# Mixer kernel on one core: plain blocks with units held in SBUF for the first supergroup

## What is computed

```python
q_s = exp(q - max(q, -1)); q_s /= sum(q_s, -1) + 1e-9
k_s = exp(k - max(k, 2));  k_s /= sum(k_s, 2) + 1e-9
x = q_s @ (k_s^T @ v)                    # to [8, 576, 512]
u = x + (relu(x^T @ w_tok1) @ w_tok2)^T
y = u + relu(u @ w_ch1) @ w_ch2          # first mixer, hidden 1536
xn = (y - mean(y)) / sqrt(var(y) + 1e-6) * g_ln
out = y + relu(xn @ w_ch1') @ w_ch2'     # second mixer, hidden 2048
```

## Time and profile before

| | us |
|---|---|
| median of 3 runs | 1565.05 (1563.29 to 1566.54) |
| profiled execution | 1563.69 |
| its span | 1561.9 |

### The profile page before, as it was taken

The page is one execution under the profiler, slowest core; times in us unless marked ns, Lnnn a source line. Parts: engine busy times, 40 slices in busy tenths (PEclk is TensorE's granted clock), DMA queues, the critical chain, the costliest instruction groups (busy, mean ns, idle before and its releaser), DMA issues.

```text
span 1561.9 us, 19837 instructions
## 1 busy us (share of the span) xinstructions
PE 1472.2 (94%) x7584; PEld 1322.4 (85%) x7584; DVE 1076.6 (69%) x1165; ACT 698.2 (45%) x844; POOL 309.0 (20%) x315
## 2 busy tenths in 40 slices
PE   6999896898999999899989999999999999999998
PEld 5988885787888887788878888888888888889998
DVE  7987876397486486496696687568657856872276
ACT  5656654352453453352452453344345424532342
POOL 6587785323303312300000000000000000000000
PEclk9999998899999999999999999999999999999999
DMA  7899985989989989979658767766876687667766
GB/s 241 256 306 296 299 282 202 403 318 366 354 291 379 372 294 362 352 288 317 240 184 300 248 209 266 249 247 219 275 243 228 237 277 244 211 219 256 251 214 199
DMA packets 150334, 429.28 MB, mean 275 GB/s; under 512 B 14240, under 2 KB 43488, under 8 KB 150240
## 3 DMA queue, kind: packets, MB, share of 16 engines
q1 hardware_dynamic: 132768, 361.94, 67.6%
q0 software_dynamic: 17472, 66.07, 11.8%
HBM read 348.26 MB, written 79.69 MB: 274 GB/s over the span
## 4 chain that ended last, share of the span: by engine, by line
PE 74%; DMA 10%; DVE 7%; issue 3%; SPq 2%; POOL 2%; ACT 2%; DVEq 0%; ACTq 0%; POOLq 0%
PE ps L1131 24%; PE ps L1133 23%; PE ps L1132 23%; DMA w_ring<-w_scratch_B 6%; DMA vt<-v 2%; SPq L289 2%; DMA qt<-q 1%; DVE o_lo L980 1%; DVE x_lo L834 1%; PE ps L1155 1%; DMA w_op<-w2b 1%; PE ps L1166 1%; DVE q_sum L761 1%; POOL q_lo L464 0%; DVE h L950 0%
## 5 line engine op out<-in xcount | busy, mean ns | idle before, releaser
L1131 PE MATMUL ps<-x_hi,w_ring 128*128 128x462 f32 (+1 forms) x980 | 369.2, 377 | 44.1 <-issue 15.1
L1131 PE MATMUL ps<-o_hi,w_ring 128*128 128x462 f32 (+1 forms) x980 | 367.4, 375 | 9.6 <-DVE o_lo L980 7.9
L1133 PE MATMUL ps<-x_hi,w_ring 128*128 128x462 f32 (+1 forms) x980 | 366.7, 374 | 0.0
L1132 PE MATMUL ps<-x_lo,w_ring 128*128 128x462 f32 (+1 forms) x980 | 366.7, 374 | 0.0
L1132 PE MATMUL ps<-o_lo,w_ring 128*128 128x462 f32 (+1 forms) x980 | 364.8, 372 | 0.0
L1133 PE MATMUL ps<-o_hi,w_ring 128*128 128x462 f32 (+1 forms) x980 | 364.6, 372 | 0.0
L671 ACT CAST o_hi<-h 128x924 fp32r<-128x924 f32 (+1 forms) x210 | 202.3, 963 | 254.8 <-PE ps L1133 225.0
L980 DVE TENSOR_TENSOR o_lo<-h,o_hi 128x924 fp32r<-128x924 f32 (+1 forms) x210 | 240.8, 1150 | 61.2 <-ACT o_hi L671 61.2
L1131 PEld LDWEIGHTS ps<-x_hi,w_ring 128*128 128x128 f32 x980 | 186.2, 190 | 74.3 <-issue 31.2
L1131 PEld LDWEIGHTS ps<-o_hi,w_ring 128*128 128x128 f32 x980 | 185.1, 189 | 40.1 <-issue 17.5
L950 DVE TENSOR_TENSOR h<-ps,h 128x924 f32<-128x924 f32 (+1 forms) x90 | 100.6, 1117 | 163.5 <-PE ps L1133 163.1
(11 more groups left out here) (140 smaller groups left out, 1831.3 us busy)
## 6 DMA issues: line engine op xcount, KB each, us to landing
w_ring<-w_scratch_C SPq DMA_DIRECT2D x280, 512.0 KB, 3.8
w_ring<-w_scratch_B SPq DMA_DIRECT2D x210, 512.0 KB, 5.6
w_scratch_C<-w_out POOLq DMA_DIRECT2D x8, 1792.0 KB, 11.7
w_scratch_C<-last_pair POOLq DMA_DIRECT2D x8, 1792.0 KB, 11.8
w_scratch_B<-w_out POOLq DMA_DIRECT2D x6, 1792.0 KB, 10.4
w_scratch_B<-last_pair POOLq DMA_DIRECT2D x6, 1792.0 KB, 9.9
kt<-kT SPq DMA_DIRECT2D x32, 288.0 KB, 6.0
u_scratch<-u_out SPq DMA_DIRECT2D x32, 288.0 KB, 3.8
```

Of the source, the lines that this page charges most:

```text
L1131: mm(dst, a_hi, b_hi, start=start, stop=False, skip_group_check=onto)
L1132: mm(dst, a_hi, b_lo, start=False, stop=False, skip_group_check=onto)
L1133: return mm(dst, a_lo, b_hi, start=False, stop=stop, skip_group_check=onto)
```

## The change

Position 0 no longer goes through `CALLS`. It is computed with plain blocks (eight products in place of seven) straight from the units that lie in SBUF: the raw blocks of a unit, with high and low part, are weights of position 0, and its four sums are made alongside and stored with them for the later positions. One raw block (the one that isn't among the seven operands) uses the last slot of the ring. TensorE works through 12 units of 48 matrix products: four groups of 12, each group with two PSUM banks. The takes, now with the relu in them, are on ScalarE after every second unit; the result is added at the end (`plain_add`). In the first stage no unit is made: two are loaded in steps 5 and 6, their raw parts cast at the end of steps 6 and 7. Low parts of all units are VectorE's. x of position 0 needs four pairs of parts and no sums. Ring entries are loaded from position 1 on. Units 13 to 27 are made at five entries in each of positions 1 to 3.

```diff
-    for pos in range(NX):
+    for pos in range(1, NX):
...
+    PLAIN = UNITS["B"]
+    HI_AT = {s * ENTRIES["B"] + e: PLAIN + 1 + 5 * s + i for s in range(3) for i, e in enumerate((0, 6, 11, 27, 36))}
...
+            w_out1 = sb("w_out1", [P, 7, 2, 2 * P], f32r, w)
...
+                if n == RW - 1:
+                    sp.wait_ge(groups, unit_over(PLAIN - 1))
...
-            for n in range(RW):
-                load_entry(n)
             step(NB - 1, 0)
             phase_a_over(sp)
+            for c in range(NC):
+                load_x(1, c)
+            for c in range(NC):
+                load_res(0, c)
+            for n in range(RW - 1):
+                load_entry(n)
+            for c in range(NC):
+                load_x(2, c)
+            store_plain(0)
+            store_plain(1)
+            load_entry(RW - 1)
+            store_plain(2)
+            store_plain(3)
...
                 if first:
                     sub_q(1, ST)
                     lo_q(1)
-                    load_unit(0)
                     return
-                load_unit(i)
+                if i in (NB - 3, NB - 2):
+                    load_unit(i - (NB - 3))
                 if later:
                     sub_q(i + 1, ST)
-                sum_unit(i - 1)
-                if later:
                     lo_q(i + 1)
-                lo_unit(i - 1)
-                store_unit(i - 1)
+                else:
+                    sum_unit(0)
+                    sum_unit(1)
...
+            for n in range(PLAIN):
+                if n >= 2:
+                    sum_unit(n)
+                store_unit(n)
+                load_unit(n + 2)
...
+            def hi_px(c):
+
+                if c == 0:
+                    act.wait_ge(kv_done, NB)
+                    act.wait_ge(x_in, 64)
+                n = 2 * SIZES[0]
+                nc.scalar.copy(plain_x(c)[0], xn[:, c * n:(c + 1) * n].rearrange("p (h n) -> p h n", h=2))\
+                  .then_inc(px_hi_made, 1)
+
+            def hi_raw(n):
+
+                act.wait_ge(wp_in[n % 2], 32 * (n // 2 + 1))
+                wait(act, wp_stored[n % 2], 16 * (n // 2))
+                if n >= 2:
+                    act.wait_ge(groups, unit_over(n - 2))
+                x = w_op[:, n % 2, :, :]
+                nc.scalar.copy(w_out[n % 2][:, 0, 0, :], x[:, 0, :]).then_inc(raw_hi_made, 1)
+                nc.scalar.copy(plain_w(n, 0, 1)[:, 0, :], x[:, 7, :]).then_inc(raw_hi_made, 1)
+                nc.scalar.copy(w_out[n % 2][:, 5:7, 0, :], x[:, 5:7, :]).then_inc(raw_hi_made, 1)
...
+            def plain(n):
+
+                if 2 <= n + 1 < PLAIN:
+                    hi_raw(n + 1)
+                if n < HC["B"]:
+                    if n % 2 == 1:
+                        plain_take(n, 0)
+                    hi_sums(n + 1)
+                    if n == 4:
+                        hi_po(0)
+                        hi_po(1)
+                    if n % 2 == 1:
+                        for g in range(1, NC):
+                            plain_take(n, g)
+                    return
+                r = 2 * (n - HC["B"]) + 2
+                if r < 2 * HC["B"]:
+                    hi_po(r)
+                if n + 1 < PLAIN:
+                    hi_sums(n + 1)
+                else:
+                    hi_unit(PLAIN)
+                if r < 2 * HC["B"]:
+                    hi_po(r + 1)
+                for p in {7: (0, 1), 8: (2, 3), 9: (4, 5), 10: (6,)}.get(n, ()):
+                    hi_x(1, p)
...
+            def plain_in(n):
+
+                pe.wait_ge(raw_lo_made, 3 * (n + 1))
+                if n == 0:
+                    pe.wait_ge(px_lo_made, NC)
+                for g in range(NC):
+                    if n == 0 and g == 1:
+                        pe.wait_ge(u_act, U_ACT * NB)
+                        pe.wait_ge(u_dve, U_DVE * NB)
+                    if n >= 2 and n % 2 == 0:
+                        pe.wait_ge(plain_relu, NC * (n // 2 - 1) + g + 1)
+                    for i in range(2):
+                        x = plain_product(plain_w(n, i, g // 2), g % 2, g, *plain_x(2 * i + n % 2),
+                                          n % 2 == 0 and i == 0, n % 2 == 1 and i == 1)
+                    x.then_inc(groups, 1)
...
+            for n in range(HC["B"]):
+                plain_in(n)
+            for n in range(HC["B"], PLAIN):
+                plain_out_of(n)
```

More of the change, by code:

```diff
@@ L624, in step @@
                             hi_q(i + 1, ST[c - 1:c])
-                    if later == 0 and c == 0:
-                        hi_x(0, 1)
+                    if later == 0 and c < 2:
+                        hi_px(2 + c)
                 if later:
                     hi_q(i + 1, ST[3:])
-                if later and not first:
-                    hi_unit(i - 1)
+                if later == 1:
+                    hi_raw(0)
+                    hi_raw(1)
             exp_q(0, ST)
@@ L691, in norm @@
                       .then_inc(root_made, 1)
-            hi_unit(NB - 2)
-            for p in (2, 3):
-                hi_x(0, p)
-            hi_unit(NB - 1)
+            hi_sums(0)
+            for n in range(PLAIN):
+                plain(n)
             for c in CALLS:
@@ new lines, in plain_add, with plain @@
+            def plain_add(g):
+                n = SIZES[0]
+                y = halves(res, n)[:, g, :, :]
+                if g == 0:
+                    dve.wait_ge(res_in, 64)
+                dve.wait_ge(groups, added(2 * HC["B"] - 1, g))
+                nc.vector.tensor_tensor(y, plain_group(g), y, ALU.add).then_inc(plain_out, 1)
+            def plain(n):
+                if 2 <= n + 1 < PLAIN:
+                    lo_raw(n + 1)
+                if n == 4:
+                    lo_po(0)
+                    lo_po(1)
+                r = 2 * (n - HC["B"]) + 2
+                if 2 <= r < 2 * HC["B"]:
+                    lo_po(r)
+                if n + 1 < PLAIN:
+                    lo_sums(n + 1)
+                else:
+                    lo_unit(PLAIN, 0)
+                    lo_unit(PLAIN, 1)
+                if 2 <= r < 2 * HC["B"]:
+                    lo_po(r + 1)
+                if n == 6:
+                    sum_x(1, 0)
+                if n == 7:
+                    lo_x(1, 0)
+                    lo_x(1, 1)
+                    sum_x(1, 1)
+                if n == 8:
+                    lo_x(1, 2)
+                    sum_x(1, 2)
+                    lo_x(1, 3)
+                if n == 9:
+                    lo_x(1, 4)
+                    lo_x(1, 5)
+                    sum_x(1, 3)
+                if n == 10:
+                    lo_x(1, 6)
@@ L941, in _ @@
             nc.vector.tensor_scalar(g_half[:, :], gcol[:, :], -0.5, None, ALU.mult).then_inc(ghalf_made, 1)
+            lo_sums(0)
+            for n in range(PLAIN):
+                plain(n)
+            for g in range(NC):
+                plain_add(g)
             def take(c, p):
```

177 lines of the change are left out of this document (118 added, 59 removed).

## The result

| | before | after |
|---|---|---|
| median of the runs | 1565.05 us (1559.63 to 1567.92) | 1555.24 us (1551.93 to 1557.58) |
| ratio | | 0.9948 (95% interval 0.9924 to 0.9972) |
| profiled execution, its span | 1563.69, 1561.9 | 1557.58, 1555.8 |

The changed kernel is faster by 0.5%, 9.8 us by the medians. The forecast was 20 us: the sign and the range held, the time that was named did not. The profiled execution of after is the slowest of its five; its gain over the profiled one of before is 6.1 us.

The account below looks back on a forecast made before the run. TensorE bounds the kernel (95% busy from 387 us), but position 0 loses time to waits and slow clock. Terms -5.0 + 0.6 - 20.5 + 2 + 1 + 2 + 1 = -18.9 took 1563.7 to 1544.8, given as 1545 us; range 1534 to 1557.

Parts of the forecast that it names:

- (1): Position 0's products: 576 plain ones at 0.2134 us take 122.9 us against 143.42, old waits gone: -20.5 us.
- (2): Start of position 0: last low part of x follows VectorE's copy, first product at about 244.1: +0.6 us (0 to +3).
- (3): Unit supply during position 0: a chain of up to 20.5 us is hidden; only the start is tight: +2 us (0 to 8).
- (4): VectorE in position 0: heaviest units hold 8.4 of 10.24 us, next x has slack: costed at nothing.
- the tight place: Start of position 0: unit 2, loaded from about 248.3, ready at 264 and wanted at 264.6; 2 us taken.
- rival D: Unit supply in position 0: 20 us from load issue to landing, 13.7 us a unit, whole slower at 1577 us; chance 0.07.
- Rivals B: Unit supply sets position 0 mildly: loads land only after stores, 12.0 us a unit, 1560 us (half effect 1552); chance 0.11.
- E: Start of position 0: first waits move rather than vanish if unit 2 comes 10 us late, 1555 us; chance 0.07.
- C: VectorE becomes position 0's bound, held up by GpSimd's sums: units 7 to 9 take 11.4 us, whole 1550; chance 0.05.
- (6): First stage without unit work: five steps come down to the 27.57 us one without a store: -5.0 us (0 to -10.7).
- rival A: First stage gains nothing: waits for v turn into waits for q's low part on GpSimd, 1550 us; chance 0.12.
- (5): Change to position 1 and after: late entry 3 +1, four y stores in position 1 +2, position 3's five units +1.

Follow-up runs that it names:

- a_work: Changed kernel with the units' sums, casts and low parts put back into its first stage, without their memory traffic: 1568.85 us, ratio 1.0006 to the kernel before.
- y_spread: Changed kernel with ring entry 3 ahead of position 0's y stores, which go one by one behind entries 5 to 8: 1553.28 us, 0.9901 of the kernel before.
- unit_late: Changed kernel with position 1's units made at entries 6, 11, 20, 27, 36 instead of 0, 6, 11, 27, 36: 1556.34 us, 0.9938 of the kernel before.
- y_late: Changed kernel with both y_spread's moved y stores and unit_late's later units: 1547.15 us, 0.9880 of the kernel before.
- b_nostore: Kernel before with the 1.8 MB stores of units 2 to 5 in first-stage steps 3 to 6 cut to 64 KB each: 1560.55 us, 0.9958.
- f1: y_spread with position 1's units at entries 5, 10, 15, 27, 36: 1548.91 us, 0.9891 of the kernel before.
- f2: As f1, but unit 12 moved to entry 3 of position 1 and the others at 8, 13, 18, 28, 37: 1551.58 us, 0.9877 of the kernel before.
- after_again: The changed kernel itself, unaltered, run once more on one chip with f1 and f2: 1556.30 us, 0.9916 of the kernel before.
- a_traffic: Changed kernel with the units' loads and 1.8 MB transfers put back into its first stage, without sums or casts: 1583.21 us, 1.0093 of the kernel before.

## Why the prediction was right or wrong

**(1) The products of position 0: right.** The sum had 122.9 us for 576 products. 355.02 - 228.28 = 126.74, less the waits of 2.73 at unit 2 and 1.09 at position 1, is 122.92. The pace of stage C held for plain blocks, the clock was 0.99, and the old waits of 10.18 and 7.82 us are gone, as forecast.

**(2) Start, (3) supply of units, (4) VectorE: right in size, except for a wait ahead of position 0.** The only wait inside position 0 is the one that was called the tight place, 2.73 us where 2 stood. Loads of units, from issue to landing, in the stretch 204 to 256 and then 256 to 345 us of after:

```profile
DMA to landing us min/median/max: 11.3/15.6/21.2
```

```profile
DMA to landing us min/median/max: 7.6/7.8/11.6
```

The load of unit 2 went out at 231.91, 3.6 us behind the first product (the sum had 4.2), and GpSimd's sums could start at 248.33: a landing of 16.4 us where 13.3 was the worst that the sum allowed. The sum had 0.6 us to spare there; the 3.1 us more of the landing, and casts and low parts of 3.1 us where it had 2.4, less the 0.6 by which the load went out earlier, come to about the 2.7. Unit 3's loads reached even the 20 us of rival D (19.8 and 21.2), but only they did: unit 4's took 11.3 to 11.6, unit 5's up to 8.7, the later ones 7.6 to 8.2. Rivals B and D, which needed slow landings in every unit, fell with that row, and so did E: unit 2 was late by 2.7 us, not 10. C fell too, though its premise held. By groups of VectorE's instructions in position 0 of after:

```profile
L967 DVE TENSOR_TENSOR w_out<-w_op,w_out 128x512 fp32r<-128x512 f32 x24 | 15.4, 686 | 15.9 <-ACT w_out L612 15.9
...
L961 DVE TENSOR_TENSOR w_out<-w_op,w_out 128x512 fp32r<-128x512 f32 x10 | 11.7, 1167 | 0.0
L959 DVE TENSOR_TENSOR w_ring<-w_op,w_ring 128x256 fp32r<-128x256 f32 x10 | 9.4, 942 | 0.0
L957 DVE TENSOR_TENSOR w_out<-w_op,w_out 128x256 fp32r<-128x256 f32 x10 | 7.7, 766 | 28.1 <-ACT w_out L606 28.1
```

The same 512 columns take 686 ns when GpSimd is done with its sums and 1167 when it sums beside them; 256 columns take 766 and 942 where the earlier trace rows has 0.42 us. The three raw parts of a unit cost 2.9 us, not 1.5. The Trainium skill (SBUF — State Buffer, Who interferes with whom) says that a VectorE instruction with two inputs in SBUF contends with a GpSimd instruction that reads SBUF; these rows agree in kind. But 1.4 us more a unit is half of the 3.0 of GpSimd's sums, which rival C added whole. Mostly this stayed hidden, with VectorE busy for 73.2 of 127 us, but not everywhere. At unit 2 the raw low parts took from 248.71 to 251.33, 2.6 us instead of 1.5, all of it in the chain that TensorE waited for: by estimate 1.1 us of the 2.7. And the sum of part (2) priced the raw parts of unit 0, in the last step but one, at nothing for VectorE: they took 3.6 us (204.02 to 207.57), a row of 512 columns 1.78, and TensorE then waited 2.40 us for qT_lo at 209.98, where the kernel before has such a wait of 1.20.

**(6) The first stage: right in sign, too small by a factor of three.** The first product came at 228.28, 15.3 us earlier; the sum had -5.0 + 0.6. The step that failed is the reference: "if the five steps come down to the one without a store". That step, 27.57 us, had no store, but it had the loads of two units, the four sums of one and its cast in it (the low parts followed at 80.91), and a DMA share of 0.84. It is not the step without a unit, which takes 25.69 us with TensorE busy for 127.13 of 128. Work (0.95) and stores (1.1 to 2.4) each had their price. The five steps that the sum counted took 207.50 - 76.58 = 130.92 us, 12.0 less than 142.88 where it had 5.0; the step ahead of them, which the sum left out, took 25.45 instead of 27.57, 2.1 less; and from the last k_den row to the first product it was 1.2 less where the sum had 0.6 more. The other reason was rival A's, which held the gain down: GpSimd's low part of q would be late next. But GpSimd had lost its own work, 68.06 us busy in 128 where it had been 112.87 in 144, and TensorE's wait for it was 0.7 us, once, against 5.2 in a_work, where that work is back. I priced the resource that was freed as though it were still loaded. Even the bound of -10.7 was passed, since it added up only waits that had been named in the stretch.

**(5) The change to position 1: wrong, and the largest error.** +3 us in the sum, up to 8.5 by its bounds, 14.8 measured. The parts were all seen: four y stores in position 1, entry 3 late behind two of them, a DMA share of 0.92. The step that failed is the price of the ring entries: each part was priced alone, the bytes at the position's mean rate and entry 3 by the 3.5 us wait that the kernel before has at this change. The store of unit 12 and of the unit of entry 0, which now fall there too, had no term. All of it falls into the same 25 us, at the one point where the ring has three entries and no more to follow. There the landing of an entry rose to 13.6 us against 7.7 us of work in the ring, and two waits with a stretch at clock 0.80 followed. y_spread, unit_late and y_late show that cause for the mixing-in half, 11.7 of the 14.8 us: either edit gives back a part, both give back the whole of that half. The other 3.1 us, in the mixing-out half, are no more than b_nostore has there (59.1 us) on the schedule of the kernel before.

**Positions 2 to 4.** Position 3 had +1; 118.2 and 115.1 against 113.6 contain it. The 4 us of position 2 weren't foreseen, came in both executions, and are unexplained: b_nostore, whose schedule there is that of the kernel before, has 118.2 as well.

**The sum.** The range held by luck. -15.3 and -16.7 against forecasts of -4.4 and -18.5 (its -20.5 and 2), then +14.8 against +3, and +11.0 in positions 2 to 4 (+5.5 in the second execution) against +1. The two large errors, 11 us too little gained and 12 too little given back, nearly cancel; what is left between 18.9 and the 6.1 us of the profiled executions is mostly positions 2 to 4, which no experiment explains.

**A better version.** The orders with the burst taken apart run at 0.988 to 0.989 of the kernel before (y_late, f1, f2), against 0.9948 and 0.9916 in the two measurements of the changed kernel. That both are beaten is likely, not shown: where they ran together the intervals still overlap, and in the profiled executions positions 1 to 3 together took 367.2 us in y_late, 364.2 in f1 and 362.3 in f2, against 366.5 in after and 363.2 in after_again. There position 2 was longer than in after (123.4, 122.5 and 120.7 against 118.9) by much of what position 1 had gained.

## What to carry to other kernels

When work leaves a stage, price what is left with everything of it gone, not by a step that lacks one part of it; and if the stage then has one engine at 99%, its end comes from that engine's own work. When a stage ends earlier or its last transfers move, list by time what is issued in the first tens of microseconds of the next one: transfers that are cheap by their bytes are dear where the prefetch has no lead. And when such a list is spread, look at what each moved piece brings along on the other engines: a unit at entry 20 took its bytes out of the burst and put its low parts ahead of what TensorE wanted next.

## What was unexpected of the hardware

At the same 400 GB/s, entries of 512 KB landed in 7.0 us in one order and in 13.6 in another. A load of 256 KB took 7.8 us in quiet stretches and up to 21.2 at the start of position 0. A VectorE operation on 924 columns that takes 1.11 us took 3.43 in y_late while GpSimd made four sums. The mixing-in half of position 1 took 66.8 to 74.5 us in four executions with the same schedule in that half (after, after_again, a_work, a_traffic, each with another history), and position 3 took 118.2 and 115.1 us in two executions of the same kernel: one profile can't settle less than that.
